# Placeholder matmuls in three TensorE waits, an expert's first weights behind three semaphores, and GpSimd's constants moved to the last chunk

## Time and profile before

| | |
|---|---|
| Median of 3 runs | 785.16 us (784.6 to 786.09) |
| Profiled execution | 785.32 us, of which its span is 783.2 us |
| PE busy | 734.6 us (94% of the span), 5911 instructions |
| PE weight loads busy | 689.5 us (88%) |
| DVE busy | 571.9 us (73%), 1458 instructions |
| ACT busy | 322.7 us (41%), 775 instructions |
| POOL busy | 153.8 us (20%), 246 instructions |
| Chain that ended last | PE 85%, DVE 6%, issue 3%, ACT 2%, DMA 1% |

### The profile page before, as it was taken

One profiled execution on the slowest core, in us unless ns is written; L12 is line 12 of the kernel. 1 busy time (PEld: TensorE's weight loads), 2 busy tenths in 40 slices (PEclk: granted clock), 3 DMA queues, 4 the chain that ended last, 5 costly groups with the idle time before them and its releaser, 6 DMA issues.

```text
span 783.2 us, 17825 instructions
## 1 busy us (share of the span) xinstructions
PE 734.6 (94%) x5911; PEld 689.5 (88%) x5911; DVE 571.9 (73%) x1458; ACT 322.7 (41%) x775; POOL 153.8 (20%) x246
## 2 busy tenths in 40 slices
PE   5999999853999999999999999999999999999994
PEld 4899999742989988998999899889989998999994
DVE  7778888977677868776877778677868777783442
ACT  5666777302234513532361245134413522361431
POOL 6367787401000110110011001101100110011001
PEclk9999999955899999999999999999999999999998
DMA  6888886104104100500320041005001400410000
GB/s 160 251 227 237 224 229 179 42 12 138 42 1 149 31 26 4 175 26 0 88 90 25 0 147 30 25 0 163 31 9 52 125 25 0 142 36 25 1 1 26
DMA packets 66781, 62.54 MB, mean 80 GB/s; under 512 B 35004, under 2 KB 57916, under 8 KB 66748
## 3 DMA queue, kind: packets, MB, share of 16 engines
q1 hardware_dynamic: 57016, 48.66, 21.8%
q0 software_dynamic: 2688, 8.65, 3.5%
q10 hardware_dynamic: 7044, 4.79, 2.0%
HBM read 53.43 MB, written 8.65 MB: 79 GB/s over the span
## 4 chain that ended last, share of the span: by engine, by line
PE 85%; DVE 6%; issue 3%; ACT 2%; DMA 1%; ACTq 1%; POOL 0%; SPq 0%; DVEq 0%
PE bank L924 21%; PE bank L930 18%; PE bank L929 18%; PE bank L948 5%; PE bank L949 4%; PE bank L800 4%; PE bank L783 2%; PE bank L751 2%; PE bank L734 2%; PE bank L974 1%; PE bank L839 1%; PE bank L973 1%; ACT decay L1079 1%; PE bank L848 1%; PE bank L918 1%
## 5 line engine op out<-in xcount | busy, mean ns | idle before, releaser
L924 PE MATMUL bank<-wo_hi,h_hi 128*128 128x320 f32 x384 | 120.6, 314 | 0.0
L930 PE MATMUL bank<-wo_hi,h_lo 128*128 128x320 f32 x384 | 118.6, 309 | 0.0
L929 PE MATMUL bank<-wo_lo,h_hi 128*128 128x320 f32 x384 | 118.0, 307 | 0.0
L1627 DVE SCALAR_TENSOR_TENSOR g_act<-g_neg,rest_alpha,bank 128x384 f32<-128x384 f32 x128 | 78.4, 613 | 40.2 <-ACT g_neg L1161 38.1
L658 POOL DMA_INDIRECT xe<-x_rows,idx_in x24 | 27.0, 1127 | 398.8 <-DVE idx_in L1565 357.7
L1161 ACT ACTIVATE g_neg<-bank 128x384 f32<-128x384 f32 x128 | 62.6, 489 | 94.9 <-PE bank L949 94.9
L1165 ACT CAST h_hi<-g_act 128x384 fp32r<-128x384 f32 x128 | 65.8, 514 | 83.7 <-DVE g_act L1627 83.2
L1159 ACT ACTIVATE h_hi<-bank 128x384 fp32r<-128x384 f32 x64 | 31.5, 492 | 162.3 <-PE bank L949 157.0
L924 PE MATMUL bank<-yT_hi,wi_hi 128*128 128x384 f32 x256 | 92.1, 360 | 0.0
L1632 DVE TENSOR_TENSOR h_lo<-g_act,h_hi 128x384 fp32r<-128x384 f32 x128 | 71.2, 556 | 26.2 <-ACT h_hi L1165 22.5
L929 PE MATMUL bank<-yT_lo,wi_hi 128*128 128x384 f32 x240 | 81.3, 339 | 0.0
(11 more groups left out here) (247 smaller groups left out, 1740.5 us busy)
## 6 DMA issues: line engine op xcount, KB each, us to landing
s<-w SPq DMA_DIRECT2D x8, 1024.0 KB, 5.2
s<-w SPq DMA_DIRECT2D x16, 480.0 KB, 7.2
s<-w SPq DMA_DIRECT2D x16, 256.0 KB, 6.0
k_in<-kT SPq DMA_DIRECT2D x48, 80.0 KB
q_in<-qT SPq DMA_DIRECT2D x48, 80.0 KB
k_row<-k SPq DMA_DIRECT2D x24, 160.0 KB, 3.4
v_in<-v SPq DMA_DIRECT2D x24, 160.0 KB, 3.9
gate_o<-o SPq DMA_DIRECT2D x24, 160.0 KB, 3.3
```

The costliest lines, as they stand in the source:

```text
L924: pe.matmul(acc, ah, bh, start=start, stop=False, skip_group_check=True)
L929: pe.matmul(acc, ah, bl, start=False, stop=False, skip_group_check=True)
L930: return pe.matmul(acc, al, bh, start=False, stop=stop, skip_group_check=True)
L1627: dve.scalar_tensor_tensor(out=g_act[:, n, :], in0=g_neg[:, :], scalar=rest_alpha[:, j:j + 1], in1=acc, op0=ALU.mult, op1=ALU.add).then_in ...
```

## The change

- **Fillers.** A new PE helper `keep_busy(n, dst)` issues n matmuls of the fp32 identity with itself into a bank that nobody reads. 14 of them stand before `turn_gates(0)`; 5, 2 and 2 around the tail steps after the last attention tile; 12 before the first gathered rows are transposed, 3 before the second and 3 before the third block of rows, and 2 before the first expert's first `up`.
- **First weights.** w1's three blocks get a transfer and a semaphore each (the third block has two transfers on one), and ACT's `high_w1` waits for its own block. That holds for all experts.
- **Constants.** `search_consts` moves from tile 1 to tile 21, `mask_consts` from tile 21 to tile 22, `routing_consts` from tile 0 to behind tile 23, before `list_consts`. `consts` counts one more, and the waits change with it.
- **Gates.** `aT` has a semaphore of its own, raised after the first of the three copies; ACT's decays wait for that. `split_peak(1)` stands behind the probabilities of tile 1.
- **Third highs.** In `up`, the matmul with the third block's highs waits only for the highs, and the waits for the lows and the second copy stand before the last matmul.
- **`add_four`** of an expert's seventh step stands one matmul earlier.
- **ACT** does `activate(0, 0)` before `high_w2(0, 1)`.

```diff
@@ load_weights
-                sp.dma_start(s1[:, 0:2, :], w1[w, 0:2 * P, :].rearrange("(t p) f -> p t f", p=P)).then_inc(stage1_in, 16)
-                sp.dma_start(s1[0:REST, 2, :], w1[w, 2 * P:DM, :]).then_inc(stage1_in, 16)
-                sp.dma_start(s1[REST:P, 2, :], w1[w, 2 * P:DM, :]).then_inc(stage1_in, 16)
+                for t in range(2):
+                    sp.dma_start(s1[:, t, :], w1[w, P * t:P * t + P, :]).then_inc(stage1_in[t], 16)
+                sp.dma_start(s1[0:REST, 2, :], w1[w, 2 * P:DM, :]).then_inc(stage1_in[2], 16)
+                sp.dma_start(s1[REST:P, 2, :], w1[w, 2 * P:DM, :]).then_inc(stage1_in[2], 16)
@@ gpsimd
-            weigh_values(0, 0)
-            routing_consts()
-            weigh_values(0, 1)
-            search_consts()
-            weigh_values(0, 2)
-            weigh_values(0, 3)
+            for b in range(B):
+                weigh_values(0, b)
...
             for b in range(1, B):
                 weigh_values(NCH - 1, b)
                 if b == 1:
+                    search_consts()
+                if b == 2:
                     mask_consts()
+            routing_consts()
             list_consts()
@@ tensor
+            def keep_busy(n, dst):
+
+                for _ in range(n):
+                    pe.matmul(dst[:, 0:P], ident[:, :], ident[:, :], start=True, stop=True)
+
+            keep_busy(14, XTB)
             turn_gates(0)
...
                 if isinstance(T, int) and T >= NT:
+                    keep_busy(5 if T == NT else 2, SCORE[0])
                     pe.wait_ge(out_read, NT)
                     pe.wait_ge(logit_read, T - 2)
                     router(*prev(c, b, 2))
+                if isinstance(T, int) and T == NT:
+                    keep_busy(2, SCORE[0])
...
-            pe.wait_ge(consts, 5)
+            pe.wait_ge(consts, 7)
...
+                keep_busy(12, UP[2])
                 for m in range(CT):
+                    if m:
+                        keep_busy(3, UP[2])
                     pe.wait_ge(first_rows[m], 16)
@@ parts3
                 pe.matmul(acc, ah, bl, start=False, stop=False, skip_group_check=True)
+                if between:
+                    add_four(*between)
                 return pe.matmul(acc, al, bh, start=False, stop=stop, skip_group_check=True)
@@ up
                 if ready:
+                    pe.wait_ge(ready if highs is None else highs, count + 3)
+                pe.matmul(acc, wh[:, 2, js], ah[:, 2, :], start=False, stop=False, skip_group_check=True)
+                if highs is not None:
                     pe.wait_ge(ready, count + 3)
                 if ready is y_ready:
                     pe.wait_ge(y_twice, count // 3 + 1)
-                pe.matmul(acc, wh[:, 2, js], ah[:, 2, :], start=False, stop=False, skip_group_check=True)
@@ tensor, before the first expert
             turn_first()
+            keep_busy(2, UP[2])
             pe.wait_ge(prep_lo, 3 * PREP + 4)
@@ scalar
-                    act.wait_ge(gates_ready, c + 1)
+                    act.wait_ge(bias_ready, c + 1)
...
-                if t == 0:
-                    act.wait_ge(stage1_in, 48 * e + 48)
+                act.wait_ge(stage1_in[t], 16 * e + 16 if t < 2 else 32 * e + 32)
...
             high_w2(0, 0)
+            activate(0, 0)
             high_w2(0, 1)
-            activate(0, 0)
             high_w2(0, 2)
@@ vector
                     ins = dve.tensor_copy(dst[:, cs, :].rearrange("p c h -> p (c h)"), GATES[i][:, 0:n])
+                    if i == 0:
+                        ins.then_inc(bias_ready, len(GROUPS[g]))
...
                 if first(T, B):
+                    if b == 0:
+                        split_peak(1)
...
             gate_peaks(1)
-            split_peak(1)
             over_chunks(dve, step, tail=(0, 1))
```

More of the change, by code:

```diff
@@ L281, in build_program @@
         gates_ready = sem("gates_ready")
+        bias_ready = sem("bias_ready")
         qk_in = [sem(f"qk_in{b}") for b in range(B)]
@@ L322, in build_program @@
         token_sum = sem("token_sum")
-        stage1_in = sem("stage1_in")
+        stage1_in = [sem(f"stage1_in{t}") for t in range(3)]
         stage2_in = [sem(f"stage2_in{t}") for t in range(3)]
@@ L575, in routing_consts @@
                 pool.iota(route_tie[:, :, :], pattern=[[-8 * P, NCH], [-8 * S, B], [-1, E]], base=8 * 4095 + E - 1, channel_multiplier=-8,
-                          allow_small_or_imprecise_dtypes=True)
+                          allow_small_or_imprecise_dtypes=True).then_inc(consts, 1)
             def search_consts():
@@ L919, in turn_rows, with parts3 @@
                 ins.then_inc(xe_turned, 1)
-            def parts3(acc, a, b, start, stop, low=None):
+            def parts3(acc, a, b, start, stop, low=None, between=None):
                 (ah, al), (bh, bl) = a, b
@@ L970, in down1 @@
                             ins = parts3(ACC[t][:, 0:CAP], (w2_hi[:, j, ds], w2_lo[:, j, ds]),
-                                         (h_hi[:, j % 3, :], h_lo[:, j % 3, :]), j == 0, j == J1 - 1)
+                                         (h_hi[:, j % 3, :], h_lo[:, j % 3, :]), j == 0, j == J1 - 1,
+                                         between=(ph, J1 - 2) if route and j == J1 - 1 and t == 0 else None)
                         else:
@@ L977, in down1 @@
                             ins.then_inc(y_acc, 1)
-                        if route and j == J1 - 1 and t == 0:
-                            add_four(ph, J1 - 2)
                     if route and j == J1 - 1:
@@ L1351, in early_bests @@
                 ch = early
+                dve.wait_ge(consts, 7)
                 ch.link(dve.tensor_reduce(row_ones[:, :], ident[:, :].rearrange("p (c r) -> p r c", r=QR), X, ALU.add))
@@ L1587, in _ @@
             match_rows(ch, 0)
-            dve.wait_ge(consts, 7)
+            dve.wait_ge(consts, 8)
             own_list(ch, 0)
```

## The result

| | us |
|---|---|
| Before, median of 4 runs beside it | 785.48 (784.6 to 786.09) |
| After, median of 4 runs | 780.67 (780.43 to 780.78) |
| Ratio | 0.9942, 95% interval 0.9928 to 0.9955 |
| Profiled execution after | 780.73, of which its span is 778.9 |
| Forecast | 782.0, range 779.6 to 784.4 |

The account below looks back on a forecast made before the run. PE was taken as full from 27.3 to 147.9 and 200.0 to 773.3, waiting elsewhere. Start 1.5 - last chunk 0.2 + first expert 1.0 + middles 0.8 = 3.1 us, giving 782.0 us, range 779.6 to 784.4.

Parts of the forecast that it names:

- The start: Up to the fades' product: 1.5 us won, ends 0.3 and 2.3.
- DVE's 2.0: At the start: DVE's chain to the fades' product gets 2.0 us shorter through earlier probabilities, later split and faster norm.
- the bound of 17.7: At the start: SP's query transfer keeps tile 2's scores from beginning before about 17.7, limiting the gain to 1.2 us.
- The last chunk: Moved constants, last tiles to first search: 0.2 us lost, bounds a gain of 0.4 and a loss of 1.5.
- of this chain's meetings one exists before: Last chunk: a DVE copy of 31 columns already took 0.61 us beside a GpSimd select, so 0.2 loss was taken.
- The first expert: Before the first `down1`: earlier weights and a higher clock start it 1.0 us earlier, ends 0.4 and 1.2.
- doesn't eat the gain: First expert: the second `down1`, held by DVE to 202.1, would start at 202.6 and leave the 1.0 us gain whole.
- The middles: Eight expert middles: third highs fill a wait, 0.17 us each, 1.4; less moved `add_four`, 0.8 taken, ends 0.2 and 1.4.
- the clock did not stay high through the search: Rival: the clock stays high in the search, nine rounds win 0.1 each, 781.1 us; chance 0.06.
- GpSimd did not stop DVE by 1.5: Rival: behind the last tile GpSimd's moved constants stop DVE, loss 1.5, time 783.4 us; chance 0.07.
- transfers did not hold every tile: Rival: transfers hold the first chunk, the start wins only 0.3, time 783.3 us; chance 0.14.
- fillers lifted the clock in both places: Opposing rival: fillers don't lift the clock and outlast their waits, mainly at the first expert, 787.0 us; chance 0.07.

Follow-up runs that it names:

- e2: Changed kernel with GpSimd's three groups of constants back where they stood before, in the first chunk and behind tile 21: 781.56 us.
- the repetition: The changed kernel run once more without any edit, as a yardstick: 780.74 us.
- e5: Changed kernel with group 1's peak split before tile 1's probabilities again: 780.84 us.
- e7: Changed kernel with `add_four` of the seventh step back behind the third matmul: 780.77 us.
- e1: Changed kernel without the 14 fillers ahead of the first gate transposes: 781.23 us.
- e10: Changed kernel with routing constants moved behind tile 21's mask and the first list mask behind tile 22's, in GpSimd's idle times: 780.62 us.
- e8: Changed kernel without the 5, 2 and 2 fillers around the last tiles: 780.79 us.
- e6: Changed kernel with w1's first two blocks in one transfer again and one semaphore for all of w1: 780.6 us.
- e3: Changed kernel without the fillers before and between the first expert's transposes (12, 3, 3, 2): 780.99 us.
- e4: Changed kernel with the third block's highs in `up` waiting for the lows and the second copy again: 782.66 us.
- e9: Changed kernel with SP's three small transfers (gate weights, alpha) moved behind tile 2's queries: 780.67 us.
- e11: Changed kernel with the edits of e9 and e10 together: 780.71 us.

## Why the prediction was right, and where it was off

**The start** was -1.67 against -1.5. The reason for cutting DVE's 2.0 to 1.5 was a right one: the bound of 17.7 for tile 2's scores was seen at 17.55, released by the transfer, and in all nine other executions with fillers and the same order of loads at 17.0 to 17.8. In eight of these nine and in the kernel after (all but e2) the fades' product follows tile 2's scores by 6.97 to 7.06 us, and in three of them DVE even waits for PE at tile 1's output (0.40, 1.04 and 0.77 us in the repetition, e5 and e7).

But DVE's chain was not 2.0 shorter either, and that two errors in it cancel in part is luck. Tile 0's result starts at 17.39 against 17.95, 0.56 earlier where 1.5 was forecast: the scans of group 1 end at 11.79, not 11.35, since they wait 0.30 for their own transfer and one takes 0.87 beside GpSimd's product, so the first probabilities end at 13.10, not 12.65; `neg_peak` took 0.81 instead of 0.34; and the split behind tile 1's probabilities did not run at 0.23 to 0.29 a part, it met GpSimd's mask (15.53 to 16.76) and its second part took 0.62. Behind tile 0's result 1.10 was won where 0.55 was forecast: besides tile 0's norm, tile 1's `nq` and norm went from 0.63 and 0.67 to 0.26 and 0.17. In all DVE's chain is 1.66 shorter (diagonal at 25.61 and 23.95), as much as the product. The fillers ended at 8.73, not 8.3, and so held the gates by up to 0.3 in that execution; the 28 took anything from 4.8 to 6.3 us over the runs. Of the parts, the order on DVE and the constants bring 1.26, the fillers 0.4 (e1), the place of the split nothing (e5). The semaphore of `aT` alone, and ACT's order before the first expert, were never undone by themselves.

**The last chunk** lost 0.54 against 0.2, the step "of this chain's meetings one exists before". It exchanged one meeting of 0.44 us for three of 0.31. I had set the conversions aside as short; they are single-input operations from SBUF to SBUF, and the three that began while a select ran were caught: they end at 148.80, 149.75 and 150.48, each 0.09 us behind the end of a select. The two-input product between them kept its 0.33, but it began beside a memset, before the next select. The conversions at 149.68 and 150.41, which began just before and just behind a select, kept their 0.22. e10 shows the cause: with the selects elsewhere all are back at 0.24. The Trainium skill (SBUF — State Buffer, Who interferes with whom) says that casts and tensor_scalars in a two-port mode and GpSimd hold each other off for a whole instruction; here the three tensor_scalars agree, at 0.31 us a meeting. By that rule alone I had put the loss near 1.5, and it was 0.54: the loss is set by how many operations of that kind begin while GpSimd is at work, not by GpSimd's moved time.

**The tail's fillers** at 0: right (e8). **The search** unchanged at 22.93: right, at a granted clock of 0.50.

**The first expert**, -1.11 against -1.0. The first `up` came 0.27 earlier relative to the list, not 0.47, the third gather's rows were transposed 8.06 behind the list, as before (8.00); the clock did the rest, `up` to `down1` 4.11 against 4.95. Two statements in it don't hold. That w1's split is what wins the earlier start was right, but it is worth nothing at the end of the stretch, where w2's way through ACT and DVE ends later (e6). And "doesn't eat the gain" was wrong for the fillers: without them the first `down1` is 1.04 later and the last product only 0.6 (e3).

**The middles** were the term that was mis-sized: 0.8 taken, 1.3 measured (e4), near the upper end of 1.4. (The table's row has 1.08; by e3, up to 0.4 that the earlier first expert gives back lies in the same stretch.) What I subtracted, 0.07 to 0.1 for the moved `add_four` in seven middles, does not exist (e7). The step I missed: the third low doesn't hang on y's first block. From ACT's first high to the end of the third low it is 2.28 us in e7 (365.20 to 367.48) and 2.17 in the kernel after (364.83 to 367.00): a first block that comes 0.1 later only shortens the waits for the blocks behind it.

**What no term held.** "From 27.3 to 147.9 ... nothing off PE can shorten these" was wrong by 0.9 us. ACT's and SP's queues of the kernel before, issues in the attention stretch:

```profile
30.13 1.63 ACTq L1095 DMA_DIRECT2D x_rows<-x_sb  x1
30.41 1.37 SPq L445 DMA_DIRECT2D k_in<-kT  x2
41.38 1.39 ACTq L1095 DMA_DIRECT2D x_rows<-x_sb  x1
41.49 1.30 SPq L445 DMA_DIRECT2D k_in<-kT  x2
```

An issue takes ACT 0.35 to 0.45 us in most places. Where it took 1.39, ACT's decays came late, PE waited at 47.59 and 49.00, and two output products lie 6.87 us apart instead of 5.94. In the kernel after no issue on ACT is longer than 0.6 us in this stretch, and the distances there stay within 6.25. This is a draw of the execution rather than the change: the stretch took 122.8 to 122.9 us in after, its repetition, e3 and e8; 123.1 to 123.5 in e1, e4, e5, e6, e7 and e9, each with one ACT issue of 0.8 to 1.2 us near 45; 123.5 in e10 and e11, with one of 0.8 to 0.9 and 0.33 from late constants; and 125.3 in e2, with one of 1.41 and the stretch at the lower clock. The long issue at 30.13 cost PE 0.2 at most (6.01 from one output product to the next instead of 5.84), one of 1.18 at 28.26 in the repetition nothing. But the kernel before also scatters more (783.7 to 788.6 over the runs here, against 780.4 to 781.5 after), so a part of the median's gain may be that it is hit more often.

The 25 runs of the kernel before that stand beside the experiments point at a second draw, TensorE's clock. Their times go with the mean granted clock: 783.7 and 783.8 us at 0.971, 784.2 to 785.4 in the eight at 0.968 (mean 784.8), 785.6 to 786.9 in the ten at 0.966 (mean 786.4), 788.6 at 0.964, and the other four between 785.2 and 786.9. An estimate from these: 0.002 less over 783 us is some 3 us more at half rate, worth up to 1.6 us, which is the distance of the two means and what the lower level cost in e2. None of the 25 is kept as a trace (the one that is, 785.32 us, has 0.968), so where they lost it is not shown. What makes the issues long, what lowers the clock, and whether the constants in the first chunk have a share in either, as e2's spread of 2.9 us would let one suspect, stays open. So do the 0.29 us around the span, which every one of the changed kernels gained (1.8 against 2.1 to 2.2).

One sum of the prediction is off: the ends of its four terms give 779.9 to 785.8, not 780 to 784. The narrower range holds only if they do not all fall to one side.

The rivals: the clock did not stay high through the search, GpSimd did not stop DVE by 1.5, transfers did not hold every tile, and fillers lifted the clock in both places, at the start with up to 0.3 us past the wait, and nothing behind them came late for it.

## What to carry to other kernels

Before valuing a saving at the place where it acts, find the next chain that ends there: at the start two chains end within some tenths of a microsecond, before the first `down1` w2's chain hides w1's, and behind it 0.4 of a saved microsecond is given back; three of the ten parts (the split of w1, the place of `split_peak`, the tail's fillers) bring nothing for this reason, and a fourth, the place of `add_four`, brings nothing either (e7). When an estimate comes out, check its steps all the same: at the start DVE's chain came out near its sum by two errors, of 0.9 and 0.55, that cancel in part. The cheapest edit brought as much as any: a wait put one matmul later, in a part that runs eight times. And when work is moved on GpSimd, look at which single-input SBUF to SBUF operations of DVE it will lie beside, one by one, and which of them begin while GpSimd's instruction runs.

## What was not expected of the hardware

- The same 28 filler instructions, from the same 2.71 us on, took 4.76 to 6.30 us in the twelve executions that have them: the moment at which TensorE goes from its lower to its upper level differs by more than a microsecond between executions. The Trainium skill (TensorE: Matmul & The Clock Gate, What's actually happening) says that the number of slow matmuls at the start varies from run to run; the trace agrees.
- The column of the granted clock says 1.00 for the first stretch in every run, though the first products ran at half rate (2.04 us against 1.16). Before the first change of level the column told nothing in these traces; durations did.
- In one profiled execution of fourteen (e2's) TensorE stood at the lower level from about 27.5 to 30.9, in the middle of dense work, and lost 1.6 us. PE had waited 0.85 us at 17.77 and 0.65 at 25.47; the kernel before had waits as long (0.69 at 18.08, 0.88 at 26.20) and stayed at the upper level.
- An issue on ACT's queue took 1.1 to 1.6 us instead of 0.35 to 0.45, in several executions while SP was issuing as well (30.13 and 30.41, 41.38 and 41.49), and its engine stood still for it.
